# An expert kernel's first rows: turned and split before a block's end instead of behind it

## What is computed

```python
for b in range(B):
    prev_e = -1
    for s in range(S):
        fresh_e = int(np.argmax(logits[b, s]))
        e = fresh_e if s == 0 or local_gate[b, s] < 0.5 or prev_e < 0 else prev_e
        prev_e = e
        ...
        h = np.maximum(x[b, s] @ w1[e], 0.0)
        out[b, s] = p[e] * (h @ w2[e])
```

## Time and profile before

| | |
|---|---|
| median of 3 runs | 680.24 us (679.5 to 680.84) |
| the profiled execution | 679.24 us, its span 677.2 us |
| mean granted clock of TensorE | 0.982 |
| PE busy | 631.4 us (93% of the span) |
| DVE, ACT, POOL busy | 399.6, 354.5, 252.3 us |

### The profile page before, as it was taken

The page is one execution under the profiler, slowest core; times in us unless marked ns, Lnnn a source line. Parts: engine busy times, 40 slices in busy tenths (PEclk is TensorE's granted clock), DMA queues, the critical chain, the costliest instruction groups (busy, mean ns, idle before and its releaser), DMA issues. The chain is left out here.

```text
span 677.2 us, 10666 instructions
## 1 busy us (share of the span) xinstructions
PE 631.4 (93%) x3792; PEld 499.9 (74%) x3793; DVE 399.6 (59%) x729; ACT 354.5 (52%) x534; POOL 252.3 (37%) x207
## 2 busy tenths in 40 slices
PE   3899999999999996699999999999779999989998
PEld 1666667667666664589799889989657888878886
DVE  6767878777877754762644345332369687542422
ACT  3776777776776774343565355332278585320200
POOL 5753718163443000286742563360476342000000
PEclk9999999999999999699999999999799999989999
DMA  9203351708183911196976665510544011422101
GB/s 297 93 1 93 149 168 75 249 17 265 40 288 84 392 64 36 59 366 237 399 263 230 248 215 191 215 63 6 175 163 139 2 44 61 145 94 68 72 32 62
DMA packets 57276, 99.18 MB, mean 146 GB/s; under 512 B 17040, under 2 KB 23184, under 8 KB 57232
## 3 DMA queue, kind: packets, MB, share of 16 engines
q1 hardware_dynamic: 54704, 90.47, 39.0%
q0 software_dynamic: 2240, 7.34, 3.2%
q10 hardware_dynamic: 288, 0.79, 0.3%
HBM read 69.23 MB, written 29.36 MB: 146 GB/s over the span
## 5 line engine op out<-in xcount | busy, mean ns | idle before, releaser
L405 DVE TENSOR_REDUCE scores<-scores 128x1 f32<-128x768 f32 x96 | 92.8, 966 | 40.5 <-PE scores L523 39.2
L346 ACT COPY probs_t<-turned 128x768 f32<-128x768 f32 x96 | 76.6, 798 | 59.9 <-PE turned L532 59.6
L354 ACT ACTIVATE probs<-scores,bias,scale 128x768 f32<-128x768 f32 x96 | 95.4, 994 | 13.2 <-DVE bias L412 12.6
L967 POOL TENSOR_TENSOR w_lo<-stage,w_hi 128x1024 fp32r<-128x1024 f32 x28 | 76.6, 2769 | 66.8 <-ACT w_hi L962 62.3
L532 PE MATMUL turned<-ident,probs 128*128 128x128 f32 x576 | 80.3, 276 | 5.2 <-ACT probs_t L346 5.2
L532 PEld LDWEIGHTS turned<-ident,probs 128*128 128x128 f32 x576 | 67.9, 142 | 14.5 <-issue 11.7
L1086 PE MATMUL up<-xt_hi,w_hi 128*128 128x256 f32 x256 | 72.4, 283 | 1.3 <-DVE xt_lo L1026 1.3
L1086 PE MATMUL up<-xt_lo,w_hi 128*128 128x256 f32 x256 | 72.3, 282 | 0.0
L1086 PE MATMUL up<-xt_hi,w_lo 128*128 128x256 f32 x256 | 72.3, 282 | 0.0
L544 PE MATMUL pv<-probs_t,v_in 128*64 128x384 f32 x384 | 72.1, 498 | 0.0
L523 PE MATMUL scores<-k_aug,q_aug 76*128 76x384 f32 x192 | 60.2, 395 | 7.5 <-DVE k_aug L398 5.1
(11 more groups left out here) (189 smaller groups left out, 1232.4 us busy)
## 6 DMA issues: line engine op xcount, KB each, us to landing
stage<-in_w SPq DMA_DIRECT2D x64, 512.0 KB, 4.2
x_slots<-zeros SPq DMA_DIRECT2D x7, 1024.0 KB, 9.4
y_slots<-zeros SPq DMA_DIRECT2D x7, 1024.0 KB, 11.5
wt_raw<-in_w_tok SPq DMA_DIRECT2D x9, 768.0 KB
q_raw<-in_qT SPq DMA_DIRECT2D x16, 384.0 KB, 5.5
k_raw<-in_kT SPq DMA_DIRECT2D x14, 384.0 KB, 6.3
x_in<-x_slots SPq DMA_DIRECT2D x8, 512.0 KB, 5.5
y_slots<-y_out SPq DMA_DIRECT2D x16, 256.0 KB, 4.6
```

The costliest lines, as they stand in the source:

```text
L346: nc.scalar.copy(probs_t[j % 2][:, a, :, t % 3 * P:(t % 3 + 1) * P].rearrange("k (b n) q -> k b n q", b=2), turned[:, :, 0:HALF].rearrange ...
L354: nc.scalar.activation(probs[g % 3][:].rearrange("p (b n) -> p b n", b=2), scores[g % 2][:, :, 0:HALF], ACT.Exp, bias=bias[:, pair, a, t:t ...
L405: nc.vector.tensor_reduce(neg_max[g % 2], scores[g % 2][:, :, 0:HALF], AX.XY, ALU.max, negate=True).then_inc(s_neg, 1)
L967: name.tensor_tensor(w_lo[w][:, r, :], stage[:, r, :], w_hi[w][:, r, :].bitcast(F32), ALU.subtract).then_inc(done, 1)
```

## The change

- `WARM_UP` becomes 48 and `EARLY_PIECES` 4.
- The buffers `xt_ps`, `xt_hi`, `xt_lo` and their semaphores are made ahead of the routing block.
- On TensorE in `routing`: 48 warm-ups, a wait for the first gather, 4 transposes, 16 warm-ups, a wait for the second gather, 4 transposes, 16 warm-ups.
- `xt_hi` of the first unit is the last thing on ScalarE in `routing`, `xt_lo` the last on VectorE there, behind the low part of piece 3.
- In `experts` the prologues of TensorE (8 transposes, 12 warm-ups) and ScalarE are empty, and VectorE's has pieces 4 to 7 alone.

```diff
-WARM_UP = 72
-
-EARLY_PIECES = 3
+WARM_UP = 48
+
+EARLY_PIECES = 4
...
+def turn_rows(nc, xt_ps, x_in, ident, half):
+    for k in range(KD):
+        last = nc.tensor.transpose(xt_ps[k // 2][:, k % 2, half * P:(half + 1) * P], x_in[:, half, k * P:(k + 1) * P],
+                                   ident[:])
+    return last
+
+
+def rows_high(nc, act, turned_rows, g):
+    xt_ps, xt_hi, _, s_xt, s_xh, _ = turned_rows
+    act.wait_ge(s_xt, g + 1)
+    for n in range(2):
+        nc.scalar.copy(xt_hi[:, 2 * n:2 * n + 2, :], xt_ps[n][:]).then_inc(s_xh, 1)
+
+
+def rows_low(nc, dve, turned_rows, g):
+    xt_ps, xt_hi, xt_lo, _, s_xh, s_xl = turned_rows
+    for n in range(2):
+        dve.wait_ge(s_xh, 2 * g + n + 1)
+        at = slice(2 * n, 2 * n + 2)
+        nc.vector.tensor_tensor(xt_lo[:, at, :], xt_ps[n][:], xt_hi[:, at, :].bitcast(F32),
+                                ALU.subtract).then_inc(s_xl, 1)
...
         for r in range(1, NP):
             piece_high(r)
+        rows_high(nc, act, turned_rows, 0)
...
                                     ALU.subtract).then_inc(s_wlv, 1)
+        rows_low(nc, dve, turned_rows, 0)
...
-        for n in range(WARM_UP):
-            nc.tensor.matmul(banks[:, 3, 0:P], route.ident_b[:], route.ident_b[:], start=True, stop=True)
+        def keep_clock(times):
+            for n in range(times):
+                nc.tensor.matmul(banks[:, 3, 0:P], route.ident_b[:], route.ident_b[:], start=True, stop=True)
+
+        xt_ps, _, _, s_xt, _, _ = turned_rows
+        keep_clock(WARM_UP)
+        for half in range(2):
+            pe.wait_ge(s_xin0[half], 16)
+            last = turn_rows(nc, xt_ps, x_in, ident, half)
+            if half == 0:
+                keep_clock(16)
+        last.then_inc(s_xt, 1)
+        keep_clock(16)
...
     @block.scalar
     def _(act):
-        def x_high(g):
-            act.wait_ge(s_xt, g + 1)
-            for n in range(2):
-                nc.scalar.copy(xt_hi[:, 2 * n:2 * n + 2, :], xt_ps[n][:]).then_inc(s_xh, 1)
-
         def prologue():
-            x_high(0)
+            pass
...
             for r in range(EARLY_PIECES, NP):
-                if r == NP // 2:
-                    x_low(0)
                 dve.wait_ge(s_wh, r + 1)
...
-        def prologue():
-            transpose_x(0)
-            keep_clock(12)
```

More of the change, by code:

```diff
@@ L642, in expert_weights, with rows_turned @@
     return stage, w_hi, w_lo, s_st, s_wh, s_wlv, s_wlp
+def rows_turned(nc, ctx):
+    xt_ps = [ctx.enter_context(nc.psum_tensor(f"xt_ps{n}", [P, 2, UNIT], F32)) for n in range(2)]
+    xt_hi, xt_lo = [ctx.enter_context(nc.sbuf_tensor(f"xt_{n}", [P, KD, UNIT], F32R)) for n in ("hi", "lo")]
+    return xt_ps, xt_hi, xt_lo, *[ctx.enter_context(nc.semaphore(f"e_{n}")) for n in ("xt", "xh", "xl")]
+def turn_rows(nc, xt_ps, x_in, ident, half):
[15 more added lines that the diff above has]
+                                ALU.subtract).then_inc(s_xl, 1)
 def load_piece(sp, w1, w2, stage, s_st, e, r):
@@ L654, in load_piece, with routing @@
     sp.dma_start(dst, src).then_inc(s_st[r], 16)
-def routing(nc, ctx, route, w1, w2, x_rows, s_rows, x_in, s_xin0, first, s_first, pos, gate, chunk_tab, weights):
+def routing(nc, ctx, route, w1, w2, x_rows, s_rows, x_in, s_xin0, turned_rows, ident, first, s_first, pos, gate, chunk_tab, weights):
     def sb(name, shape, dt=F32):
@@ L853, in _, with experts @@
         last.then_inc(s_tok, 1)
-        for n in range(WARM_UP):
-            nc.tensor.matmul(banks[:, 3, 0:P], route.ident_b[:], route.ident_b[:], start=True, stop=True)
+        def keep_clock(times):
[10 more added lines that the diff above has]
+        keep_clock(16)
 KF = F // P
-def experts(nc, ctx, w1, w2, x_all, x_rows, x_in, s_xin0, first, s_first, y_out, pos, x_slots, s_clear, y_slots, ident, ident_b, chunk_tab, weights, load_theta):
+def experts(nc, ctx, w1, w2, x_all, x_rows, x_in, turned_rows, first, s_first, y_out, pos, x_slots, s_clear, y_slots, ident, chunk_tab, weights, load_theta):
     def sb(name, shape, dt=F32):
@@ L873, in experts @@
     stage, w_hi, w_lo, s_st, s_wh, s_wlv, s_wlp = weights
-    xt_hi = sb("xt_hi", [P, KD, UNIT], F32R)
-    xt_lo = sb("xt_lo", [P, KD, UNIT], F32R)
+    xt_ps, xt_hi, xt_lo, s_xt, s_xh, s_xl = turned_rows
     ht_hi = sb("ht_hi", [P, KF, UNIT], F32R)
@@ L880, in experts @@
     up = [ps(f"up{n}", [P, 2, UNIT]) for n in range(4)]
-    xt_ps = [ps(f"xt_ps{n}", [P, 2, UNIT]) for n in range(2)]
     down = [ps(f"down{n}", [P, 512]) for n in range(2)]
@@ L1060, in transpose_x @@
         def transpose_x(g):
[L1061 to L1068, removed]
-            last.then_inc(s_xt, 1)
-        def keep_clock(times):
-            for n in range(times):
-                nc.tensor.matmul(down[0][:, 0:P], ident_b[:], ident_b[:], start=True, stop=True)
-        def prologue():
-            transpose_x(0)
-            keep_clock(12)
+            pe.wait_ge(s_xin, 16 * g)
+            for half in range(2):
+                last = turn_rows(nc, xt_ps, x_in, ident, half)
+            last.then_inc(s_xt, 1)
         def unit(g, e, w):
@@ L1104, in unit @@
                 last.then_inc(s_down, 1)
-        prologue()
         def one(e, w):
@@ L1587, in build @@
             weights = expert_weights(nc, tokens, stage, s_st)
+            turned_rows = rows_turned(nc, tokens)
             with ExitStack() as ctx:
-                routing(nc, ctx, route, w1, w2, x_rows, s_rows, x_in, s_xin0, first, s_first, pos, gate, chunk_tab, weights)
+                routing(nc, ctx, route, w1, w2, x_rows, s_rows, x_in, s_xin0, turned_rows, ident, first, s_first, pos,
+                        gate, chunk_tab, weights)
             routed.close()
@@ L1596, in build @@
             with ExitStack() as ctx:
-                experts(nc, ctx, w1, w2, x_all, x_rows, x_in, s_xin0, first, s_first, y_out, pos, x_slots, s_clear, y_slots, ident, ident_b, chunk_tab, weights,
+                experts(nc, ctx, w1, w2, x_all, x_rows, x_in, turned_rows, first, s_first, y_out, pos, x_slots, s_clear, y_slots, ident, chunk_tab, weights,
                         lambda sp: load_w(sp, w_raw, s_wraw, w_theta))
```

7 lines of the change are left out of this document (2 added, 5 removed).

## The result

The changed kernel took 683.4 us (median of 5 runs, 682.0 to 683.84), the kernel before 679.5 beside it (678.42 to 680.84): ratio 1.0054, 95% interval 1.0037 to 1.0070. By the ratio it is 3.7 us slower. The profiled execution took 683.84 us, the longest of the five; its span is 681.8.

A forecast was written before the change was run, and what follows sets the result against it. TensorE, busy 93% of the span, was taken as the bound, with its first product's time what the change moves: +1.7 (start) + 2.9 (clock) - 1.2 (stalls absorbed) = +3.4 us, giving 683.6 us, range 680.6 to 685.6.

The forecast's parts named there:

- The release behind VectorE's drain: Barrier ending the routing block: VectorE's drain would be last, after `xt_lo` at 287.6, releasing TensorE at 287.85 us.
- The register work is exposed: TensorE behind the barrier: 2.2 us of `chunk_tab` reads and loop set-up with nothing hiding them; first product 1.7 us later.
- Half 0 and the fourth low part are free: Routing block: turning half 0 and making one more low part (1.15 us of VectorE) would delay nobody.
- The clock falls in the gap: TensorE idle 3.7 us ahead of the first product: granted clock would fall to 0.50, costing 2.9 us.
- What is given back: First two units: stalls behind the load stream, 0.3 and 0.9 us, would be absorbed by TensorE's lateness, saving 1.2 us.
- the clock is kept: Rival, first products: clock stays up, stalls stay or grow by 0.5, +1.7 to +2.7 us, 682.4; chance 0.16.
- the stalls are not given back: Rival, first two units: transfers slip as far as TensorE does, +4.6 to +5.1 us, 685.1; chance 0.10.
- Whatever follows is shifted as a whole: Everything behind the second unit: TensorE meets no such wait there, so the rest would only move by the same delay.

The follow-up runs named there:

- run without reads: Changed kernel without TensorE's register reads of `chunk_tab`, one unit taken per expert, its loop over units left out; ratio 1.0055 to the kernel before.
- run with two passes: Changed kernel with TensorE's two reads of `chunk_tab` made twice for each expert; ratio 1.0168 to the kernel before.
- run with three low parts: Changed kernel with `EARLY_PIECES` back at 3, the fourth low part behind the barrier again; ratio 1.0053 to the kernel before.
- bridged kernel with four loads early: Changed kernel with extra warm-ups over TensorE's gap, and pieces 0 to 3 of the second expert loaded in the routing block; ratio 1.0057 to the kernel before.
- late-transfer run: Kernel before, with SyncE's loads of the second expert and GpSimd's next gathers made to wait for `xt_lo`; ratio 1.0051 to the kernel before.
- bridged kernel: Changed kernel with 32 warm-ups instead of 16 ending the routing block and 30 starting the experts' block; ratio 1.0112 to the kernel before.

## Why the prediction was right in its number, and what its reasons left out

The forecast was +3.4 us and 683.6; measured were +3.7 and 683.4. That the two times meet within 0.2 us is partly luck: the kernel before came out 0.7 lower than the 680.24 that the forecast started from. Point by point:

- *The release behind VectorE's drain.* Right: half 1 was turned by 285.95 and `xt_lo` done at 287.9, forecast 287.6, with traces 0.17 apart from the start.
- *The register work is exposed.* Right: 2.4 us for 2.3, first product +1.95 for +1.7. The run without reads brought it 1.7 earlier, the run with two passes 1.4 later.
- *Half 0 and the fourth low part are free.* Right: half 0 cost nothing, and the run with three low parts took the same time.
- *The clock falls in the gap.* It did in this execution, for 6.8 us, and cost 2.4 at the second products (forecast 2.9). But the reason given, that a gap of 3.7 is beyond all that fell, doesn't hold: with a gap of 3.71 it was kept in the run with three low parts, and it fell behind 1.81 and 1.92. In how many executions it falls isn't known from one trace.
- *What is given back.* 1.7 us instead of 1.2 in these two traces. The prediction counted the two waits for `ht_lo`; TensorE also loses 0.1 at the product behind each and some more ahead of the next unit's transposes. In the changed kernel all of it is gone, as forecast. With 4.3 - 1.7 = 2.6 us TensorE's own delay accounts for the whole of the last unit's lateness, and the bridged kernel with four loads early shows the same sum where no transfer is waited for (4.1 - 1.7 = 2.4).
- *What the sum left out.* The late transfers are a bound of their own. I asked only how much of the stalls they leave; they begin 2.7 us (loads) and 1.5 us (gathers) later behind the held barrier. Held back alone, with TensorE on time, they cost +3.4 us (+3.4 in the last unit's place too). With TensorE 2.6 us earlier at its second products and the transfers as late as in the change, nothing came back, although in that run the cause of the wait isn't named by the profile. So each of the two, taken alone, is enough for about the loss that was measured, and in the changed kernel they end the first unit at the same time (40.3 either way). No run holds TensorE back by the full 4.3 us with the barrier where it was; the bridged kernel with four loads early comes nearest. That the two bounds are equal is chance, and it is why a sum over TensorE's path alone came out right. The rival "the clock is kept" (682.4) came out otherwise for this reason: with the clock kept, in the trace of the run with three low parts, that execution took 678.6 us, 2.9 over the kernel before. It forecast stalls at most 0.5 longer, and what the late transfers alone cost is 3.4. The rival nearest to the second bound, "the stalls are not given back", saw the transfers only as an addition to TensorE's loss and stood at 685.1.
- *Whatever follows is shifted as a whole.* Wrong: from the last unit to the end the two traces part by another 1.9 us. 1.4 of it is the half clock from 497.4 to 500.8, on work that before ran at 1.00, after an idle stretch of the same length (2.25 and 2.23 us). In the late-transfer run the time's +3.4 equals the last unit's +3.4, in the changed kernel the +3.7 is 1.1 more than its +2.6. How much of the 1.1 lies in the mixing in every execution stays open; no run isolated it. Single traces and medians part by more elsewhere (+1.5 at the last unit against +3.6 in time with three low parts).

What makes TensorE's products come in bursts isn't settled either. The bridged kernel with and without early loads shows that it hangs on when the loads run; the changed kernel shows that it needs more than full DMA engines. The cause stays open.

## What to carry to other kernels

Before work is moved ahead of a barrier, look at which drain ends it, and count what every other engine starts behind it: here 1.9 us of splitting ahead of the barrier held back TensorE's register work and, by 2.7 us, the loads. If half of the work fits under the drain that is last anyway, move that half alone (ratio 0.9988, hardly to be told from no change, instead of 1.0054). And where a product stream and a load stream meet, reckon both and take the later one, instead of adding terms. It takes two runs to tell them apart, one that holds back the transfers alone and one that holds back the products alone by the full amount; when both cost the same, mending one gains nothing.

## What the runs showed of the hardware

- GpSimd's drain lasts until its gather has landed: with half 0 alone ahead of the barrier the drain ended at 284.7 and the gather had landed at 284.6; with four early loads beside it the landing was at 285.9 and the drain's end at 286.0. An indirect transfer ahead of a block's end therefore holds the barrier.
- With the DMA engines full (share 1.04), TensorE's products started in bursts 1.42 to 1.43 us apart, with no wait, in two kernels, whose second units began 5.6 and 6.9 us later than the changed kernel's. It went in the one that was also run with 2 MB of loads issued earlier. In the changed kernel, with the same share of 1.04, TensorE ran without a break.
- The length of a gap doesn't tell the clock behind it: it was 0.50 behind gaps of 1.81, 1.92 and 2.35 us, and 1.00 through one of 3.71; the same place in the mixing kept it behind 2.23 us before the change and lost it behind 2.25 after.
- A pass of two register reads with their range work took 1.4 us where nothing hid it.
